# Low parts of w_out on VectorE, work on x spread over other pairs, and two subtractions and roundings one group earlier

## The reference

```python
# x: 1536 x 512, the attention's output
for e in range(8):                      # 192 tokens each
    h = np.maximum(x[mask] @ w1[e], 0.0)    # w1: 512 x 1024
    out[mask] = h @ w2[e]                   # w2: 1024 x 512
x = out
a = x @ w_a                             # w_a, w_b: 512 x 1536
b = x @ w_b
return a * b @ w_out                    # w_out: 1536 x 512
```

## Time and profile before

| | us |
|---|---|
| median of 3 runs | 661.95 (660.35 to 662.78) |
| the profiled execution | 662.47 |
| its span, first to last instruction | 660.7 |
| PE busy | 606.7 (92% of the span) |
| DVE busy | 410.2 (62%) |
| ACT busy | 317.0 (48%) |
| POOL busy | 321.4 (49%) |
| TensorE's mean granted clock | 0.949 |

### The profile page before, as it was taken

How to read it: one execution, slowest core, us unless ns; L and a number is a source line. 1 busy time by engine, 2 the same in 40 slices (tenths; PEclk the granted TensorE clock), 3 DMA queues, 4 the chain that set the end, 5 groups by cost and what they waited for, 6 DMA issues and landing times.

```text
span 660.7 us, 10889 instructions
## 1 busy us (share of the span) xinstructions
PE 606.7 (92%) x3840; PEld 541.9 (82%) x3840; DVE 410.2 (62%) x1062; ACT 317.0 (48%) x772; POOL 321.4 (49%) x330
## 2 busy tenths in 40 slices
PE   7999999999542999999999899998999999999995
PEld 4877767776421899999999899998899999999994
DVE  3667755864575387667888365565466566656654
ACT  3576645763230376767776442552434234234310
POOL 4000000000002401225987898999986888787623
PEclk9898999999555799999999999999999999999999
DMA  9974142040401546676576033022022241311002
GB/s 189 263 156 97 49 132 69 16 138 26 152 0 33 160 162 191 223 224 222 192 255 223 33 96 96 32 65 95 34 92 69 66 157 64 97 33 33 32 1 95
DMA packets 87512, 72.07 MB, mean 109 GB/s; under 512 B 39840, under 2 KB 74656, under 8 KB 87456
## 3 DMA queue, kind: packets, MB, share of 16 engines
q1 hardware_dynamic: 85536, 65.05, 33.6%
q0 software_dynamic: 1920, 6.29, 2.9%
HBM read 65.04 MB, written 6.29 MB: 108 GB/s over the span
## 4 chain that ended last, share of the span: by engine, by line
PE 70%; POOL 14%; DVE 6%; ACT 5%; issue 3%; DMA 1%; DVEq 0%; ACTq 0%; POOLq 0%
PE psum L1774 13%; PE psum L1852 6%; PE psum L1855 6%; PE psum L1854 6%; PE psum L1775 6%; PE psum L1587 6%; POOL w_lo L715 5%; PE psum L1767 4%; PE psum L1769 4%; PE psum L1768 4%; PE psum L1565 3%; PE psum L1552 3%; PE psum L1592 2%; PE psum L1529 2%; POOL x_hl L679 2%
## 5 line engine op out<-in xcount | busy, mean ns | idle before, releaser
L715 POOL TENSOR_TENSOR w_lo<-w_raw,w_hi 128x512 fp32r<-128x512 f32 x96 | 109.3, 1174 | 21.6 <-ACT w_hi L911 21.2
L645 POOL MEMSET thr<- 128x8 f32 x1 | 0.1, 105 | 162.2 <-PE psum L1672 162.2
L1774 PE MATMUL psum<-h_hl,w_hi 128*128 128x384 f32 x256 | 75.4, 363 | 3.1 <-DVE w_lo L1021 1.8
L1774 PE MATMUL psum<-x_hl,w_hi 128*128 128x384 f32 x256 | 75.5, 366 | 1.6 <-DVE x_hl L1396 1.6
L1854 PE MATMUL psum<-x_hl,w_hi 128*128 128x384 f32 x216 | 72.3, 335 | 0.0
L801 ACT ACTIVATE w_hi<-w_raw 128x1024 fp32r<-128x1024 f32 (+1 forms) x72 | 69.0, 958 | 0.0
L1508 DVE TENSOR_TENSOR o_acc<-psum,o_acc 128x512 f32<-128x512 f32 x60 | 41.5, 692 | 40.7 <-PE psum L1769 40.7
L1775 PE MATMUL psum<-x_hl,w_lo 128*128 128x192 f32 x256 | 64.8, 253 | 0.0
L1021 DVE TENSOR_TENSOR w_lo<-w_raw,w_hi 128x1024 fp32r<-128x1024 f32 x44 | 64.8, 1472 | 0.0
L1775 PE MATMUL psum<-h_hl,w_lo 128*128 128x192 f32 x256 | 64.2, 251 | 0.0
L1852 PE MATMUL psum<-t_first,w_hi 128*128 128x384 f32 x168 | 56.8, 338 | 3.6 <-ACT w_raw L976 3.5
(11 more groups left out here) (220 smaller groups left out, 1590.8 us busy)
## 6 DMA issues: line engine op xcount, KB each, us to landing
w_raw<-in_moe_w_dram SPq DMA_DIRECT2D x32, 1024.0 KB, 5.5
w_raw<-in_moe_w_a_dram SPq DMA_DIRECT2D x12, 512.0 KB, 3.5
w_raw<-in_moe_w_b_dram SPq DMA_DIRECT2D x12, 512.0 KB, 3.6
w_raw<-in_moe_w_out_dram SPq DMA_DIRECT2D x12, 512.0 KB, 3.4
k_raw<-in_k_dram SPq DMA_DIRECT2D x16, 192.0 KB, 3.8
q_raw<-in_q_dram SPq DMA_DIRECT2D x16, 192.0 KB, 4.2
v_sb<-in_v_dram SPq DMA_DIRECT2D x16, 192.0 KB, 4.2
xs_scratch<-x_rows SPq DMA_DIRECT2D x8, 384.0 KB, 3.4
```

The lines of the kernel that those rows point to most:

```text
L715: return nc.gpsimd.tensor_tensor(out_t, t, hi_t.bitcast(f32), ALU.subtract)
L1774: nc.tensor.matmul(bk[:, 0:2 * CAP], lhs_hi, rhs_both, start=first, stop=False)
```

## The change

It has four parts.

1. split_out moves from GpSimd to VectorE, as one subtraction of 1024 columns. In factor_a(n) it stands for pair n-1 behind u3; for the last pair it stands in factor_b behind lower_b(n, 2).
2. The sums of x for the second half are made in pairs 1, 2 and 4 in place of 1, 2 and 3, their rounding and low parts in pairs 2, 3 and 5 in place of 2, 3 and 4.
3. round_t for the first half is called at group (2, 0) of experts 4 to 6 in place of (2, 1).
4. In the last expert VectorE makes the low part of unit 3 behind groups (1, 0) and (1, 1) in place of (1, 1) and (2, 0).

```diff
+        T_ADDED, T_SPLIT = (1, 2, 4), (2, 3, 5)
...
-            def split_out(n):
-                pool.wait_ge(unit_hi[2], n + 1)
-                for at in range(2):
-                    hs = slice(at * DM, (at + 1) * DM)
-                    op = nc.gpsimd.tensor_tensor(o_w[1][:, hs], raw_o[:, hs], o_w[0][:, hs].bitcast(f32),
-                                                 ALU.subtract)
-                op.then_inc(unit_lo[2], 1)
-
...
-                if 2 <= n < 2 + PIECES:
-                    split_t(1, n - 2)
-                if n == 0:
-                    split_out(0)
+                if n in T_SPLIT:
+                    split_t(1, T_SPLIT.index(n))
                 if n + 1 < STAGES:
                     add_blocks(0, n + 1)
                     split_mix(0, n + 1)
-                if n > 0:
-                    split_out(n)
-                if 1 <= n < 1 + PIECES:
-                    add_t(1, n - 1)
+                if n in T_ADDED:
+                    add_t(1, T_ADDED.index(n))
...
-                        if 4 <= e < E - 1 and (u, g) == (2, 1):
+                        if 4 <= e < E - 1 and (u, g) == (2, 0):
                             round_t(0, e - 4)
...
-                if 2 <= n < 2 + PIECES:
-                    round_t(1, n - 2)
+                if n in T_SPLIT:
+                    round_t(1, T_SPLIT.index(n))
...
-                        if e == E - 1 and (u, g) in ((1, 1), (2, 0)):
-                            split_lo(e, 3, u - 1)
+                        if e == E - 1 and u == 1:
+                            split_lo(e, 3, g)
...
+            def split_out(n):
+
+                dve.wait_ge(unit_hi[2], n + 1)
+                nc.vector.tensor_tensor(o_w[1][:], raw_o, o_w[0][:].bitcast(f32), ALU.subtract).then_inc(unit_lo[2], 1)
...
                 nc.vector.tensor_tensor(u3_sb, yb, p1_sb, ALU.add).then_inc(a_made, 1)
+                if n > 0:
+                    split_out(n - 1)
                 dve.wait_ge(products_a, 7 * n + P5)
...
                     lower_b(n, 2)
+                    split_out(n)
                 dve.wait_ge(products_b, 7 * n + P3)
```

## The result

The changed kernel takes 668.14 us, the median of 4 runs (667.01 to 671.25); the kernel before, run beside it, takes 661.29 us (4 runs, 660.35 to 662.78). The ratio is 1.0109, with the interval 1.0068 to 1.015: slower, by about 1%, and 0.2 us from the forecast of 667.9. The profiled execution took 667.62 us, with a span of 665.9.

What follows compares the result with a forecast made beforehand. TensorE, busy 92% of the span, was taken to set the pace from pair 6 on. Terms 8.9 + 1.1 - 2.4 - 0.3 - 1.5 + 0.1 = +5.9 us gave 667.9 against median 661.95; range 665.5 to 670.5.

Steps and rivals of the forecast that it cites:

- Insert, eleven times: Factor A, pairs 1 to 11: VectorE's w_out subtraction delays a22, so P3; 0.81 us a pair, +8.9 us.
- the restart: TensorE after any wait: loses 0.11 us more, its second matmul coming 0.28 us behind the first, not 0.17.
- The 0.28 us that a22 had to spare: Factor A, quiet pair: a22 ends at 582.16, P3's first matmul starts at 582.44; on this all hangs.
- Last insert: Last down, pair 11: it also waits for the insert behind the last g subtractions, until 647.16; +1.1 us.
- GpSimd's relief: Pairs 2, 3, 5: GpSimd's chain starts on time, P2 of factor B waits 0.55 us each; -2.4 us.
- 1.3 if twice as much is: P2 of factor B: bound on GpSimd's relief if twice the forecast wait is left; 1.3 us gained.
- Rounding of x (part 3): Experts 4 to 6: rounding starts 1.16 us earlier, shortening TensorE's waits for L641; -1.5 us, bounds 0 and -1.7.
- Last w2 part (part 4) and mix(0, 1): Last expert: 1.8 us wait goes, P2 of mix(0, 0) starts as now, +0.1; mix(0, 1) starts earlier, -0.3 us.
- Rival 1: Factor A: the insert fits, P3 is not held and the relief remains; -4.8 us, 657.2 us; chance 0.12.
- Rival 2: Factor A: the insert never meets a GpSimd instruction, no change; +0.5 us, 662.5 us; chance 0.15.
- rival 3: Factor A: the insert meets a long GpSimd instruction just begun; +14.6 us, 676.5 us; chance 0.07.
- GpSimd's place is tied to TensorE: Quiet pairs: ScalarE's L911, which follows TensorE, releases GpSimd's w_lo subtractions, so they stay in place against TensorE.

Runs made afterwards that it cites:

- part 1 alone: Kernel before with only its two GpSimd subtractions for w_out replaced by the VectorE insert, parts 2 to 4 left out; ratio 1.0123 against before.
- the copy first: Changed kernel with ScalarE's second rounding for mix(1, 0) put behind the copy of P1 of mix(0, 0); ratio 1.0133, four runs 664.28 to 677.52 us.
- parts 2 to 4 alone: Changed kernel with w_out's low part back on GpSimd, the call for pair 0 too; ratio 0.9962 against the kernel before, 12 runs.
- half the insert: Changed kernel with the insert making the low part of only 512 of 1024 columns, used for both blocks; one run, 662.2 us.
- only the last insert moved: Changed kernel with the last insert moved to the head of factor B of pair 11, the others where they are; one run, 667.44 us.

## Why the prediction was right, and where not

Term by term, forecast and measured:

- **Insert, eleven times**: +8.9, measured 11 x 0.78 = +8.6. P3's first matmul comes 0.83 us behind its neighbour in place of 0.17, so 0.66 late where 0.70 was forecast, and the restart adds its 0.11. The chain was the forecast one: issue behind u3, wait for GpSimd's second subtraction, 1.08 us from its end, a22 late, P3 late. The 0.28 us that a22 had to spare were the number to look at.
- **Last insert**: +1.1, measured +1.08 (17.07 to 18.15).
- **GpSimd's relief**: -2.4, measured 1.16 - 5 x 0.78 = -2.7 (119.24 - 118.08 less the five inserts between). TensorE's matmul at P2 of pairs 2, 3 and 5 comes 0.48 us behind its neighbour, 0.42 late with the restart, where 0.55 was forecast. The size is right and one step of the reason is not: the chain was to start on time because pairs 3 and 4 do fewer sums and low parts of x, but part 1 alone gives the same 119.2 us. Part 1 is enough; how much of that is GpSimd's loss of two long instructions and how much TensorE's coming 0.78 us later in each pair, no run tells apart. The bound "1.3 if twice as much is" was also added up wrongly: 4.2 less twice 1.7 is 0.8. It changes no other number.
- **Rounding of x (part 3)**: -1.5, measured -1.2 in experts 5 and 6 by their half-expert stretches (10.2, 9.11, 9.95 and 9.27 us before; 9.65, 9.1, 9.45 and 9.1 after). The last experiment makes it 0.6 at most, so this term isn't confirmed.
- **Last w2 part (part 4) and mix(0, 1)**: +0.1 - 0.3, measured -0.1 together (34.09 to 34.77 us, less 0.78 for the insert there). The statement that P2 of mix(0, 0) absorbs the gain is shown by the run without part 4.

The sum is 5.7 against 5.9, and 5.5 in the span's table; the medians differ by 6.9, with an interval (4.5 to 9.9) that takes in both. **What was missed** is the clock: 1.4 us at the last down. The forecast priced a longer idle time at its length and had nothing for what it may do to the clock behind it. In the profiled execution an early start of the experts made up for it, so that the closeness of the two totals is partly luck: the terms of the insert, not the total, bear the prediction out.

Rival 1 (the insert fits) is refuted in its place, and true of the quiet pairs one and two instructions ahead of it. Rival 2 (it never meets GpSimd) would have shown quiet pairs of 23.3, rival 3 of 24.4; the changed kernel's trace has 23.57 in each of the pairs from 6 on, and eleven inserts of 1.54 to 1.55 us. That GpSimd's place is tied to TensorE, on which the choice between them rested, holds: it begins 1.05 us ahead of u3 in both traces.

## What to carry to other kernels

A move to a faster engine is priced by its place in that engine's queue: list the instruction behind it, what waits for that, and how early it is now; where less is to spare than the added work, try the slots ahead of it first. Where two engines hold each other up for whole instructions, as VectorE and GpSimd do here, place the short, urgent work so that it begins ahead of the other's long row, and let the one with idle time wait. And when a wait is taken away, look in the queue of the next releaser for work that nobody needs yet.

## What the runs showed of the hardware

**Turns between VectorE and GpSimd.** A VectorE subtraction of two SBUF tiles that begins while GpSimd runs one ends 1.08 us after GpSimd's, in all eleven pairs of the changed kernel, and GpSimd's next one takes 2.27 us in place of 1.29. With half the columns it is 0.55 us. The Trainium skill ("SBUF — State Buffer", "SBUF: two separate sides") has an exclusive lock for a whole instruction, and the traces agree. They show beyond it that VectorE's waiting instruction goes ahead of GpSimd's next. That one begins 0.41 us after the insert in the rows, so a rule of turns and one of first come, first served would both give this; no run tells them apart. By the formula that the Trainium skill has for an fp32 addition of two tiles ("VectorE: DVE Perf Modes", the section on the TRN2 errata) the insert alone is estimated at (1024 + 151) / 0.96 GHz = 1.22 us. The insert with GpSimd idle took 1.22 us, so the trace agrees.

**The clock after an idle TensorE.** After idle times of 2.2 to 2.5 us ahead of a dense stretch the granted clock fell to 0.50 (1.2 GHz) in six cases of eleven, for 3.4 us each time, which cost 1.4 to 1.6 us: at the last down in the changed kernel, with the insert ahead of u3, and without part 4, but not with part 1 alone or with the copy first; at P2 of mix(0, 0) with parts 2 to 4 alone, with half the insert and with only the last insert moved, but not in the three others that waited there. After 1.96 us or less ahead of these stretches it did not fall in any. One such stretch, at P2 in the kernel with half the insert, after 2.16 us of idle time:

```profile
374.80:378.10 3.30, 3.26 (x10) 3.26 (x11) 0.56 (x1) 0.93 (x2) 3.16 (x4) 0.50 0.00 0
```

What decides between the cases isn't settled. Where it fell at the last down, the last insert cost 2.5 to 2.7 us and not 1.1.

**Left open.** In all six kernels of the study whose quiet pairs take 22.79 us the pair behind the sixth down, in which GpSimd issues stores, takes 23.3 to 23.8, and with part 1 alone 24.32 against 23.57; TensorE waits there for a sum of VectorE, for ScalarE's copy of P1, or for both. It is in neither of the profiles of before and after, and no run tells its cause. Nor is it known why an undelayed half-expert stretch takes 9.10 us at some times and 9.28 at others, also within one execution.
